# Moving operand transposes behind the scores, rehearsing a gather, and transposing each gathered tile once

## The reference, cut to what matters

```python
# 1. attention with a cluster mask: B 2, H 8 (16 heads), S 768, D 64, 16 clusters
mask = q_assign[:, :, :, None] == k_assign[:, :, None, :]
scores = np.where(mask, scale * q @ k.T, -1e9)
attn = softmax(scores); attn_out = attn @ v
x = attn_out.transpose(0, 2, 1, 3).reshape(1536, 512)
# 2. top-1 mixture of 8 experts, D 512, F 1024
e_idx = argmax(x @ w_gate)
for e in range(8):
    out[mask] = gate_w * sigmoid * (relu(x[mask] @ w1[e]) @ w2[e])
# 3. a dense layer 512 -> 2048 -> 512 with a clipped quadratic between
g = where(h >= 1, h, where(h <= -1, 0, (h + 1)**2 / 4)); return g @ w_out
```

## Time and profile before

| | |
|---|---|
| time, median of 3 runs | 810.23 us (809.6 to 810.27) |
| the profiled execution's own time | 811.1 us |
| its span, first to last instruction | 809.3 us |
| mean granted TensorE clock | 0.982 |
| PE busy | 781.1 us, 97% of the span |
| DVE, ACT, POOL busy | 55%, 47%, 41% |

### The profile page before, as it was taken

The page is one execution under the profiler, slowest core; times in us unless marked ns, Lnnn a source line. Parts: engine busy times, 40 slices in busy tenths (PEclk is TensorE's granted clock), DMA queues, the critical chain, the costliest instruction groups (busy, mean ns, idle before and its releaser), DMA issues.

```text
span 809.3 us, 12646 instructions
## 1 busy us (share of the span) xinstructions
PE 781.1 (97%) x4234; PEld 664.2 (82%) x4235; DVE 448.1 (55%) x794; ACT 381.1 (47%) x754; POOL 335.6 (41%) x321
## 2 busy tenths in 40 slices
PE   7899999999999759999999999999999999999996
PEld 4799999999998648888888888888888888888885
DVE  6898899889989853212222222244545444554453
ACT  4899889988997554222222232222223222332222
POOL 2346654555641068689659658664000100010001
PEclk9999999999999869999999999999999999999998
DMA  7675585658433187799769769592000100010001
GB/s 159 149 208 139 109 209 139 148 106 196 89 63 95 49 293 250 243 349 328 252 228 327 254 224 350 198 299 62 1 1 0 53 1 0 1 53 1 0 1 52
DMA packets 69426, 114.86 MB, mean 142 GB/s; under 512 B 30272, under 2 KB 33856, under 8 KB 68352
## 3 DMA queue, kind: packets, MB, share of 16 engines
q1 hardware_dynamic: 53568, 70.17, 30.6%
q0 software_dynamic: 15808, 44.04, 16.3%
HBM read 92.37 MB, written 6.29 MB: 122 GB/s over the span
## 4 chain that ended last, share of the span: by engine, by line
PE 93%; DVE 3%; ACT 1%; issue 1%; DMA 0%; POOL 0%; POOLq 0%; DVEq 0%; ACTq 0%
PE ps L1639 16%; PE ps L1593 16%; PE ps L1551 13%; PE ps L1571 13%; PE ps L1370 8%; PE ps L1356 4%; PE ps L1388 4%; PE ps L1357 4%; PE ps L1386 4%; PE ps L1400 2%; PE ps L1561 2%; PE ps L1300 2%; PE ps L1321 1%; PE ps L1524 1%; PE ps L1337 1%
## 5 line engine op out<-in xcount | busy, mean ns | idle before, releaser
L412 POOL TENSOR_TENSOR weights<-raw_w,weights 128x2048 fp32r<-128x2048 f32 x34 | 157.1, 4626 | 48.5 <-DMA weights<-in_moe_w 35.1
L1639 PE MATMUL ps<-weights,g_t 128*128 128x512 f32 x576 | 141.0, 394 | 0.3 <-DVE g_t L1222 0.3
L1593 PE MATMUL ps<-y_t,weights 128*128 128x512 f32 x564 | 136.9, 391 | 0.0
L1639 PEld LDWEIGHTS ps<-weights,g_t 128*128 128x128 f32 x576 | 107.3, 188 | 24.7 <-DVE g_t L1194 0.8
L1593 PEld LDWEIGHTS ps<-y_t,weights 128*128 128x128 f32 x564 | 105.8, 188 | 23.5 <-POOL weights L412 0.2
L1551 PE MATMUL ps<-weights,x_t 128*128 x456 | 112.2, 402 | 1.0 <-issue 1.0
L564 POOL DMA_INDIRECT out<-y_sb,order_u x12 | 11.7, 978 | 235.5 <-ACT y_sb L828 233.8
L1571 PE MATMUL ps<-weights,h_t 128*128 x456 | 109.3, 395 | 0.0
L985 DVE TENSOR_TENSOR p_t<-ps,p_t 128x384 fp32r<-128x384 f32 x192 | 97.6, 550 | 9.2 <-ACT p_t L641 8.5
L1551 PEld LDWEIGHTS ps<-weights,x_t 128*128 128x128 f32 x456 | 85.9, 192 | 19.4 <-issue 1.5
L786 ACT ACTIVATE ps<-g_a,half 128x512 f32<-128x512 f32 x47 | 32.5, 692 | 143.7 <-DVE g_b L1184 143.7
(11 more groups left out here) (191 smaller groups left out, 1024.3 us busy)
## 6 DMA issues: line engine op xcount, KB each, us to landing
raw_w<-in_moe_w SPq DMA_DIRECT2D x32, 1024.0 KB, 6.2
weights<-in_moe_w POOLq DMA_DIRECT2D x28, 1024.0 KB, 8.9
qk_t<-qk_t SPq DMA_DIRECT2D x47, 192.0 KB, 3.2
qk_t<-qk_t SPq DMA_DIRECT2D x16, 384.0 KB, 4.0
raw_w<-in_moe_w_in SPq DMA_DIRECT2D x4, 1024.0 KB, 6.2
weights<-in_moe_w_in POOLq DMA_DIRECT2D x4, 1024.0 KB, 8.4
raw_w<-in_moe_w_out SPq DMA_DIRECT2D x4, 1024.0 KB, 9.5
weights<-in_moe_w_out POOLq DMA_DIRECT2D x4, 1024.0 KB, 12.3
```

The source lines that it names most:

```text
L412: pool.tensor_tensor(weights[:, unit % 2, 1, c * CHUNK:(c + 1) * CHUNK], low_chunk(unit, c), high_chunk(unit, c).bitcast(F32), ALU.subtrac ...
L1593: last = mm(ps[:, UP_BANKS[n % 2], :], wi[:, a, k, f * P:(f + 1) * P], y_ts[g % 2][:, b, k, :], start=(k == 0 and j == 0), stop=(k == KC - ...
L1639: last = mm(ps[:, t, :], g_t[:, n % 2, a, t * P:(t + 1) * P], wo[:, b, f, :], start=(f == 0 and j == 0), stop=(f == FC2 - 1 and j == 2))
```

## The change

Three edits, in one kernel.

1. **Attention.** In slot 2 (all heads but the first) PE's order becomes probability transposes, prob_values, scores, operands, where it was transposes, operands, scores, prob_values. In slot 5 the operands go between scores and prob_values. Head 14 has no operands left; its prob_values still moves ahead of the scores in slot 2.
2. **Gather.** POOL issues one more indirect DMA before it waits for the token order. It takes its indices from the constant token numbers, goes to the last tile of `xs`, and is waited for (`rehearsed`) only before the twelfth real gather, which overwrites it.
3. **Experts.** PE transposes each of the twelve gathered tiles once (`tile_xt`, 4 transposes, into bank 4, 6 or 7), ACT puts the result back over `xs` (`keep_tile`), and each item's ACT copy moves the transposed tile from `xs` to PSUM bank 4 (`copy_tile`), from where `evac_xt` on ACT and DVE split it as before. `x_in` is gone. Tiles 0 and 1 are turned before and within hidden(0); tile i + 2 in item i, for i = 0 to 9. These ten items are now written out, and the loop runs the six of items 10 to 15.

```diff
@@ POOL
             pool.wait_ge(x_kept, 16 * 4)
+            pool.indirect_dma_start(out=xs[:, NT - 1, :], out_offset=None, in_=x_rows,
+                                    in_offset=bass.IndirectOffsetOnAxis(const_i[:, NI - NT:NI - NT + 1].bitcast(U32), 0))\
+                .then_inc(rehearsed, 16)
             pool.wait_ge(r_step, R_ORDER)
             for t in range(NT):
+                if t == NT - 1:
+                    pool.wait_ge(rehearsed, 16)
                 pool.indirect_dma_start(out=xs[:, t, :], ...
@@ ACT
-            def copy_rows(i, u):
...
-                act.activation(x_in[:, u, :], xs[:, bass.ds(t, 1), :].squeeze(1), ACT.Copy).then_inc(x_copied, 1)
+            def keep_tile(t):
+                if t == 0:
+                    act.wait_ge(xtl_done, 1)
+                else:
+                    act.wait_ge(tile_tr, t)
+                act.activation(xs[:, t, :], ps[:, TILE_BANKS[min(t, 2)], :], ACT.Copy).then_inc(tile_kept, 1)
+            def copy_tile(i, tiles):
+                act.wait_ge(tile_kept, tiles)
+                act.wait_ge(xtl_done, i)
+                t = act.value_load(table_i[0:1, 1, bass.ds(i, 1)], min_val=0, max_val=NT - 1)
+                act.activation(ps[:, 4, :], xs[:, bass.ds(t, 1), :].squeeze(1), ACT.Copy).then_inc(x_copied, 1)
...
             evac_xt(0, 0)
+            keep_tile(0)
             act.wait_ge(r_step, R_TABLE)
-            copy_rows(1, 1)
+            keep_tile(1)
+            copy_tile(1, 2)
+            evac_xt(1, 1)
             relu(0, True, (0,))
-            evac_xt(1, 1)
             cast_high(2)
             relu(0, True, (1,))
-            copy_rows(2, 0)
@@ PE, attend
-                    if s == 2 and ahead >= 2:
+                    if s == 2 and first:
                         pe.wait_ge(ohq_done, 2 * (h + 2))
                         operands(h + 2, 1, i + 1, u, (oh_done, h + 2))
+                    if s == 2 and not first and ahead:
+                        prob_values(h, s - 1, u, first)
...
-                    if s == 5 and ahead >= 3:
-                        operands(h + 3, 0, i + 1 + u, un, (cl_done, CL_PH * (h + 2) + 1))
                     if s < 2:
                         scores(h, 4 + s, u, first)
                     elif ahead >= 1:
                         scores(h + 1, s - 2, un, False)
+                    if s == 2 and ahead >= 2 and not first:
+                        pe.wait_ge(ohq_done, 2 * (h + 2))
+                        operands(h + 2, 1, i + 1, u, (oh_done, h + 2))
+                    if s == 5 and ahead >= 3:
+                        operands(h + 3, 0, i + 1 + u, un, (cl_done, CL_PH * (h + 2) + 1))
@@ PE, experts
+            def tile_xt(t):
+                pe.wait_ge(gathered[min(t, 3)], 16 if t < 3 else 16 * (NT - 3))
+                if t > 2:
+                    pe.wait_ge(tile_kept, t)
+                if t == 2:
+                    pe.wait_ge(r_step, R_LAST)
                 for n in range(KC):
-                    last = tr(ps[:, 4, n * P:(n + 1) * P], rows[:, n * P:(n + 1) * P], ident[:])
-                last.then_inc(xt_done, 1)
+                    last = tr(ps[:, TILE_BANKS[min(t, 2)], n * P:(n + 1) * P], xs[:, t, n * P:(n + 1) * P], ident[:])
+                last.then_inc(tile_tr if t else xt_done, 1)
...
                 if ahead >= 1:
                     hidden(i + 1, 1 - u, False)
-                if ahead >= 2:
-                    item_xt(i + 2, u, k + 1, False)
+                if tile:
+                    tile_xt(tile)
...
-            item(0, 0, 0, True, 3)
-            item(1, 1, 0, False, 3)
-            with pe.Fori(1, (ITEMS - 3) // 2) as k:
+            for i in range(NT - 2):
+                item(i, i % 2, i + 2, i == 0, 3)
+            with pe.Fori((NT - 2) // 2, (ITEMS - 3) // 2) as k:
```

More of the change, by code:

```diff
@@ L195, in build @@
     assert moe[0] <= nc.sbuf_usable_end
-    assert routing[0] <= moe[0]
-    kept = [max(moe[0], small[0])]
+    kept = [max(moe[0], small[0], routing[0])]
     r_d = place("r_d", [P, NT, E], F32, kept)
@@ L707, in _ @@
             cast_high(1)
-            def copy_rows(i, u):
[L711 to L714, removed]
+            def keep_tile(t):
[7 more added lines that the diff above has]
+                act.wait_ge(xtl_done, i)
                 t = act.value_load(table_i[0:1, 1, bass.ds(i, 1)], min_val=0, max_val=NT - 1)
-                act.activation(x_in[:, u, :], xs[:, bass.ds(t, 1), :].squeeze(1), ACT.Copy).then_inc(x_copied, 1)
+                act.activation(ps[:, 4, :], xs[:, bass.ds(t, 1), :].squeeze(1), ACT.Copy).then_inc(x_copied, 1)
             def evac_xt(i, u):
-                act.wait_ge(xt_done, i + 1)
+                if isinstance(i, int) and i == 0:
+                    act.wait_ge(xt_done, 1)
+                else:
+                    act.wait_ge(x_copied, i)
                 if not (isinstance(i, int) and i < 2):
@@ L745, in evac_rows, with item @@
                 act.activation(y_ts[g % 2][:, 0, k, :], ps[:, ROWS_BANKS[g][k % 2], :], ACT.Copy).then_inc(yth_done, 1)
-            def item(i, u, k, first, ahead):
+            def item(i, u, tile, first, ahead):
                 evac_ht(i, first)
@@ L758, in item @@
                     relu(i + 1, False)
-                if ahead >= 2:
+                if ahead >= 3:
+                    if tile:
+                        keep_tile(tile)
+                    copy_tile(i + 2, tile + 1 if tile else NT)
                     evac_xt(i + 2, u)
@@ L764, in item @@
                     evac_rows(0, 3)
[L765 to L766 removed]
             evac_xt(0, 0)
+            keep_tile(0)
             act.wait_ge(r_step, R_TABLE)
[L770 removed]
+            keep_tile(1)
+            copy_tile(1, 2)
+            evac_xt(1, 1)
             relu(0, True, (0,))
[L772 removed]
             cast_high(2)
             relu(0, True, (1,))
[L775 to L780 removed]
+            for i in range(NT - 2):
+                item(i, i % 2, i + 2, i == 0, 3)
+            with act.Fori((NT - 2) // 2, (ITEMS - 3) // 2) as k:
+                item(2 * k, 0, 0, False, 3)
+                item(2 * k + 1, 1, 0, False, 3)
             for i in range(ITEMS - 3, ITEMS):
[L782 removed]
+                item(i, i % 2, 0, False, ITEMS - 1 - i)
             def square(n):
@@ L1261, in _ @@
             item(1, 1, 0, False, 3)
-            with dve.Fori(1, (ITEMS - 3) // 2) as k:
+            for i in range(2, NT - 2):
+                item(i, i % 2, i // 2, False, 3)
+            with dve.Fori((NT - 2) // 2, (ITEMS - 3) // 2) as k:
                 item(2 * k, 0, k, False, 3)
@@ L1431, in attend @@
                         cluster_rows(h + 2)
-                    if s > 0 and (ahead or s != 4):
+                    if s > 0 and (ahead or s != 4) and (s != 2 or first or not ahead):
                         prob_values(h, s - 1, u, first)
@@ L1544, in hidden @@
                 for n in range(F // BANK):
-                    if first and n == 1:
-                        item_xt(1, 1, 0, False)
                     for j, (k, a, b) in enumerate(by_half if first and n == 0 else by_row):
                         if first and n == 0 and j == 2 * KC:
+                            tile_xt(1)
                             pe.wait_ge(xtl_done, 1)
@@ L1610, in item @@
                 output(i, u, unit_base(i, 1), isinstance(i, int) and i < 2)
-            item_xt(0, 0, 0, True)
+            tile_xt(0)
             hidden(0, 0, True)
             field_rows()
-            item(0, 0, 0, True, 3)
-            item(1, 1, 0, False, 3)
-            with pe.Fori(1, (ITEMS - 3) // 2) as k:
-                item(2 * k, 0, k, False, 3)
-                item(2 * k + 1, 1, k, False, 3)
+            for i in range(NT - 2):
+                item(i, i % 2, i + 2, i == 0, 3)
+            with pe.Fori((NT - 2) // 2, (ITEMS - 3) // 2) as k:
+                item(2 * k, 0, 0, False, 3)
+                item(2 * k + 1, 1, 0, False, 3)
             for i in range(ITEMS - 3, ITEMS):
-                item(i, i % 2, i // 2, False, ITEMS - 1 - i)
+                item(i, i % 2, 0, False, ITEMS - 1 - i)
             wo = weights[:, 1].rearrange("p a (k f) -> p a k f", k=FC2)
```

13 lines of the change are left out of this document (5 added, 8 removed).

## The result

The changed kernel takes 804.55 us (median of 6 runs, 803.75 to 805.86) against 810.04 us (809.6 to 810.88, 6 runs) for the kernel before: a ratio of 0.9932, with a 95% interval of 0.992 to 0.9944. That is 5.5 us less, and clear of the noise. Predicted were 804.3 us, a range of 802.8 to 807.6, and faster.

A forecast was written before the change was run, and what follows sets the result against it. PE was taken as the bound, busy 97% of the span. Terms of -3.0, -2.9 and 0 sum to -5.9 us, taking the median of 810.2 to 804.3 us; the 8 in 10 range was 802.8 to 807.6.

The forecast's parts named there:

- edit 3, seven groups: Experts: seven groups of four transposes go from PE's full path, at 0.43 us each, 3.0 us saved.
- edit 1, thirteen heads: Attention slots 2 and 5: PE's waits of 0.12 and 0.10 us vanish in 13 heads, 2.9 us saved.
- edit 2 and the handover: Routing to experts: gather 0.5 us earlier, but ACT's longer order holds the second relu; sum 0, bounds -0.6 and +0.4.
- it fits by a hair: Attention slot 4: `whole`, 0.4 us late, still serves PE's second three transposes, wanted at 161.49, with L985 ending about 161.44.
- Rival 1: Attention is held by ACT and DVE, so moving operands gives 0 to 1 us; 806.7 us; chance 0.15.
- Rival 2: Late `whole` copy makes PE wait in slot 4; gain gone from 0.45 us a head, 812.8 at 0.65; chance 0.07.
- Rival 3: Experts' gain doesn't come: a weight part or ACT fills the hole and PE waits; 807.3 us; chance 0.06.
- the tie at w_in: Last w_in load ends at 527.72, PE starts up at 527.77; both come 3 us earlier, cost nothing.
- Rival 4: Whole kernel: nothing measurable changes, Rival 1 and Rival 3 together; 809.5 us; chance 0.05.
- rival 5: Handover: the gather's 0.5 us is kept and PE's clock also returns earlier; 803 us; chance 0.07.

The follow-up runs named there:

- e7: The kernel before, with its seven loop turns over items 2 to 15 written out as straight code on PE, ACT and DVE; 810.21 us, ratio 1.0.
- e9: The changed kernel with one extra ACT copy ahead of the copy to `whole` in slot 2 of heads 1 to 13; 810.73 us, ratio 1.0008.
- e4: The changed kernel with ACT's cast_high(2) moved behind the second relu of item 0; 803.66 us, ratio 0.9918.
- e2: The kernel before with only the rehearsed gather added; 809.76 us, ratio 0.9995.
- e3: The kernel before with only the tiles transposed once and the loops as in the change; 807.77 us, ratio 0.9973.
- e10: e4 with eight filler matmuls into an unused bank behind PE's order matmuls; 803.08 us, ratio 0.9916.
- e8: e4 without the rehearsed gather; 803.68 us, ratio 0.9922.
- e11: The changed kernel with slot 2 in the order transposes, prob_values, operands, scores; 804.30 us, ratio 0.9926.
- e13: e11 with the extra ACT copy of e9 in slot 2; 804.46 us, ratio 0.993.
- e12: e4 with ten filler matmuls behind the order matmuls and two more between the first tile transposes and hidden(0); 807.00 us, ratio 0.9962.

## Why the prediction was right

| term | predicted | measured |
|---|---|---|
| edit 3, seven groups | -3.0 | 221.50 - 224.72 = -3.2 |
| edit 1, thirteen heads | -2.9 | -2.6 |
| edit 2 and the handover | 0 | 16.22 - 16.30 = -0.1 |
| sum | -5.9 | -5.9 in the profiles, -5.5 in the medians |

**Edit 3** was right in its mechanism and 7% small. The term was 7 x 0.43; taking the groups out shortens an item by 12.34 - 11.88 = 0.46. The chain gives a group 0.43 or 0.44 where it stands, and its removal 0.02 to 0.03 more. The Trainium skill (TensorE: Matmul & The Clock Gate, Back-to-back issue gap) gives about 81 ns a matmul at 128 columns, which would have made 2.3. Seven groups at 3.2 us are 115 ns a transpose, so the measurement decides against that figure for this instruction. ACT's added steps stayed hidden once past item 0: from hidden(3) to hidden(11), where each item still has four transposes, the distance is 12.34 to 12.35 us. The loop cost nothing, as e7 shows. The Trainium skill (Runtime: NRT & Kernel Launch, Instruction fetch mechanics) has a taken branch out of the fetched pages stall the engine, and unrolling preferred. In e7, with seven turns written out, nothing was there to win.

**Edit 1** was right in its mechanism and its size a tenth too large. From slot 4 of head 0 to slot 4 of head 13 it is 208.14 us before and 205.57 after: 2.57 saved, 0.20 a head, not 0.22. I had sized slot 2 from one head (2.51); the mean of heads 1 to 12 is 2.48. The new length of 2.39 was exact. The copy `whole` starts 157.47 - 154.82 = 2.65 us after its slot, predicted 2.6, and slot 4 did not grow; e9 shows how little stood behind the words "it fits by a hair": of 0.48 us more, 0.47 were paid. The prediction looked for that edge in the second transposes of slot 4; in e9 more than half of the loss is in slot 3, whose end waits for the copies.

**Edit 2** started the gather 0.61 us sooner and hidden(0) 0.6, where 0.5 was costed, and the second relu stood behind cast_high(2) as predicted: e4 takes 0.96 us off by moving the cast alone. The relu was forecast near 302.4 less the gain of attention, which is 299.8 with the 2.6 above; it came at 299.28, of which 0.5 is the earlier start-up. But that the term came out at nothing is in part luck. The prediction took the clock's return as it was in its one profile. There it was late (12.7 us after the order), hidden(0) ended late with it, and ACT's order had not begun to hold PE. Where the clocks came back alike (11.1 to 11.3), ACT's longer order costs 16.22 - 15.44 = 0.78 us (changed kernel against e2) and the rehearsal brings 16.83 - 16.22 = 0.61 (against e3): some 0.2 us more in all, within the stated bounds of -0.6 and +0.4.

The profiled spans differ by 809.3 - 802.8 = 6.5 us. The 0.6 beyond the sum is largely the start-up: slot 4 of head 0 begins at 34.05 before and 33.58 after, and the profile of the kernel before has a half-clock stretch of 3.4 us near 10 us, which no part of the change touches and e7's profile doesn't have. Another 0.2 is behind the first `up`. The medians, at 5.5, are nearer the sum.

**The rivals.** Rival 1 (attention held by other engines) is refuted by slots of 2.39 and 2.40. Rival 2 did not occur, but e9 makes it: `whole` 0.48 us later takes 0.47 us a head and eats the whole gain, as its price of 0.45 a head said. Rival 3 fell with items of 11.88 us and the tie at w_in moving by 6.34 us as a whole. Rival 4's time should be 810.2 - 0.5 = 809.7, not 809.5; nothing hangs on it. Of rival 5 the profile has the earlier clock (11.1 against 12.7), but no run ties it to the change; and the handover kept its length until the cast was moved.

The lowest ratios of this case are those of e10, e4 and e8, 0.9916 to 0.9922. Their intervals hold each other's ratios and overlap that of the change, so the plain exchange of e4 is the one to take, for the 0.96 us that its profile shows; whether fillers pay is open. e11's order has the same time as the change, and e13 shows that it has room for 0.48 us more on ACT, which the change hasn't.

## What to carry to other kernels

Read a wait in PE's stream by what it starts 0.14 us behind, move the waiting group behind work that is there anyway, and then price the other end: what the moved group feeds comes later (here by 0.48 us), and an extra copy of known length shows how much of that is free. Average a stall over all its repetitions before multiplying; the head that was read was 0.03 us above the mean in slot 2, which 13 heads make 0.4. When an early gain vanishes, look at the first in-order queue behind it: here the place of one cast ahead of one relu cost 0.96 us. And before two handovers are compared, put beside them when the clock came back in each; in e2's profile the clock moved the end of hidden(0) by more than the edit did.

## What was not expected of the hardware

- PE's granted clock fell twice in one handover. In the profiles of e11, e13 and e12 PE had been idle for 1.83, 2.05 and 3.77 us ahead of item_ht(0), and from 0.3 to 0.5 us behind its start 0.50 was granted for 3.4 us. With 0.37 to 1.56 us ahead of the same instruction (1.56 in e3) it stayed at 1.00.
- The same eight fillers left the clock at 0.50 in e10's profiled execution, while four of its six executions have a higher mean granted clock (0.990 and 0.992 against 0.988). In e12 the clock was back at 286.3, during the ninth filler, and the kernel was slower.
- The first gather starts 0.88 us after the order that it waits for and takes 1.05 us; after a rehearsal 0.27 and 0.98. The rehearsal itself took 1.31.
- The ninth of the twelve gathers took 2.68 us of POOL in the kernel before and 2.99 to 3.00 in all others, where most take 0.95; in ten of the fourteen profiles the twelfth took 1.94 to 2.98 too. Both were hidden, and their cause was not looked for.
